# Row maxima subtracted on GpSimd, one exponential for a group of four blocks

## What is computed

```python
k_sum = k.reshape(B, H, nb, block, D).max(axis=3)      # block = 32, nb = 24
v_sum = v.reshape(B, H, nb, block, D).mean(axis=3)
scores_l = scale * np.matmul(q, k.transpose(0, 1, 3, 2))
mask_l = np.abs(pos[:, None] - pos[None, :]) < window   # window = 16
scores_s = scale * np.einsum('bhsd,bhnd->bhsn', q, k_sum) + np.log(block)
scores_all = np.concatenate([np.where(mask_l, scores_l, -1e9), scores_s], axis=-1)
scores_all = scores_all - np.max(scores_all, axis=-1, keepdims=True)
a = np.exp(scores_all)
a = a / (np.sum(a, axis=-1, keepdims=True) + 1e-09)
attn = np.matmul(a, np.concatenate([v, v_sum], axis=2))
```

## Time and profile before

| what | value |
|---|---|
| time, median of 3 runs | 504.31 us (503.15 to 505.6) |
| span of the profiled execution | 501.4 us |
| TensorE busy | 478.4 us (95%) |
| VectorE busy | 221.7 us (44%) |
| ScalarE busy | 191.6 us (38%) |
| GpSimd busy | 114.6 us (23%) |
| TensorE busy, 30 to 60 us | 25.52 of 30 us |
| ScalarE busy, 30 to 60 us | 27.21 of 30 us |

### The profile page before, as it was taken

One profiled execution on the slowest core, in us unless ns is written; L12 is line 12 of the kernel. 1 busy time (PEld: TensorE's weight loads), 2 busy tenths in 40 slices (PEclk: granted clock), 3 DMA queues, 4 the chain that ended last, 5 costly groups with the idle time before them and its releaser, 6 DMA issues.

```text
span 501.4 us, 8399 instructions
## 1 busy us (share of the span) xinstructions
PE 478.4 (95%) x2968; PEld 444.9 (89%) x2968; DVE 221.7 (44%) x575; ACT 191.6 (38%) x424; POOL 114.6 (23%) x98
## 2 busy tenths in 40 slices
PE   4798789998999999999999999999999999999996
PEld 4677678787999999999999999999889989989985
DVE  5598887499411141114111411456436355444521
ACT  3799887424211121112111211345455256353411
POOL 6364553285999000000000024300000000000000
PEclk9999999999999999999999999999999999999999
DMA  9999997144443100000000010000010001001001
GB/s 196 181 208 215 228 213 186 46 126 129 166 149 145 43 1 0 0 0 0 0 0 0 0 42 0 0 1 0 1 49 14 0 21 42 0 0 63 0 0 63
DMA packets 48657, 31.70 MB, mean 63 GB/s; under 512 B 21248, under 2 KB 42496, under 8 KB 48640
## 3 DMA queue, kind: packets, MB, share of 16 engines
q1 hardware_dynamic: 48640, 31.49, 26.4%
HBM read 27.14 MB, written 3.15 MB: 60 GB/s over the span
## 4 chain that ended last, share of the span: by engine, by line
PE 84%; SPq 5%; DMA 5%; ACT 2%; issue 2%; DVE 1%; POOL 0%; ACTq 0%; POOLq 0%
PE bank L946 26%; PE bank L947 26%; PE bank L948 26%; DMA kn<-in_k_dram 4%; SPq L301 2%; PE bank L998 1%; SPq L310 1%; DMA v<-in_v_dram 1%; PE bank L976 1%; ACT e_sb L518 1%; PE bank L1017 1%; ACT qbd L498 1%; PE bank L895 1%; SPq L321 1%; PE bank L928 1%
## 5 line engine op out<-in xcount | busy, mean ns | idle before, releaser
L845 DVE SCALAR_TENSOR_TENSOR rL<-bank,rH 128x384 fp32r<-128x384 f32 x48 | 26.7, 557 | 148.2 <-ACT rH L614 148.2
L614 ACT ACTIVATE rH<-bank 128x384 fp32r<-128x384 f32 x48 | 23.6, 492 | 163.1 <-PE bank L948 158.7
L946 PE MATMUL bank<-uH,W1H 128*128 128x384 f32 x192 | 64.8, 337 | 0.0
L947 PE MATMUL bank<-uL,W1H 128*128 128x384 f32 x192 | 64.6, 336 | 0.0
L948 PE MATMUL bank<-uH,W1L 128*128 128x384 f32 x192 | 64.4, 336 | 0.0
L947 PE MATMUL bank<-xkL,WkH 128*128 128x384 f32 x128 | 43.3, 338 | 0.0
L946 PE MATMUL bank<-xkH,WkH 128*128 128x384 f32 x128 | 43.1, 337 | 0.0
L948 PE MATMUL bank<-xkH,WkL 128*128 128x384 f32 x128 | 42.8, 335 | 0.0
L947 PEld LDWEIGHTS bank<-uL,W1H 128*128 128x128 f32 x192 | 36.1, 188 | 0.0
L948 PEld LDWEIGHTS bank<-uH,W1L 128*128 128x128 f32 x192 | 36.0, 188 | 0.0
L946 PEld LDWEIGHTS bank<-uH,W1H 128*128 128x128 f32 x192 | 36.0, 188 | 0.0
(11 more groups left out here) (131 smaller groups left out, 1093.2 us busy)
## 6 DMA issues: line engine op xcount, KB each, us to landing
stg<-in_moe_w_ch_dram SPq DMA_DIRECT2D x12, 512.0 KB, 3.6
vw<-in_v_dram SPq DMA_DIRECT2D x16, 240.0 KB, 4.9
kn<-in_k_dram SPq DMA_DIRECT2D x16, 192.0 KB, 3.8
qn<-in_q_dram SPq DMA_DIRECT2D x16, 192.0 KB, 4.4
v<-in_v_dram SPq DMA_DIRECT2D x16, 192.0 KB, 5.1
out_dram<-o_sb SPq DMA_DIRECT2D x12, 256.0 KB, 2.0
stg<-in_moe_w_k_dram SPq DMA_DIRECT2D x4, 512.0 KB, 3.5
stg<-in_moe_w_v_dram SPq DMA_DIRECT2D x4, 512.0 KB, 3.4
```

The costliest lines, as they stand in the source:

```text
L614: act.activation(rH[f % 2][:, :], bank[f % 2][:, 0:GR], ACT.Relu).then_inc(rh_done, 1)
L845: dve.scalar_tensor_tensor(out=rL[f % 2][:, :], in0=bank[f % 2][:, 0:GR], scalar=0.0, in1=rH[f % 2][:, :].bitcast(F32), op0=ALU.max, op1=A ...
L946: pe.matmul(dst, wH, mH, start=start, stop=False, **more)
L947: pe.matmul(dst, wH, mL, start=False, stop=False, **more)
```

## The change

GpSimd gets a new operation for each group, `below_max(G, r)`: it waits for the four maxima and subtracts `nmx`, spread over the 120 columns of each block, from `s_sb` in place. It raises `sub_done`. ScalarE waits for that and takes one exponential of 480 columns, without a bias. `exp_done` counts groups now. On GpSimd the three steps of `sum_values` are spread over the three groups of a pair, each behind that group's `below_max`; `split_x` of the pair before stands in group 1 and the low half of a weight (`low_wt`) at the end of group 2. The loop over pairs is written out.

```diff
+            def below_max(G, r):
+                pool.wait_ge(max_done, GU * G + GU)
+                pool.tensor_tensor(s_sb[r][:, :, :], s_sb[r][:, :, :],
+                                   nmx[:, r, :].unsqueeze(2).to_broadcast([P, GU, COLS]),
+                                   ALU.subtract).then_inc(sub_done, 1)
...
-            def pair(p, par, i=None):
-                if i is not None:
-                    sum_values(p + 2)
...
-                split_x(p)
+            def pair(p, par, i=None, earlier=True):
+                for r in range(NG):
+                    below_max(3 * p + r + 3, r)
+                    if i is not None:
+                        sum_values(p + 2, (r,))
+                    if r == 1 and earlier:
+                        split_x(p - 1)
+                    if i is not None and r == NG - 1:
+                        low_wt(p, par, i)
...
             sum_values(0)
+            below_max(0, 0)
+            below_max(1, 1)
             sum_values(1)
-            with pool.Fori(0, NP // 2 - 1) as i:
-                for par in range(2):
-                    pair(2 * i + par, par, i)
+            below_max(2, 2)
+            for p in range(NP - 2):
+                pair(p, p % 2, p // 2, p > 0)
             pair(NP - 2, 0)
+            split_x(NP - 2)
             split_x(NP - 1)
...
             def exps(G, r, par):
-                act.wait_ge(max_done, GU * G + GU)
-                for n in range(GU):
-
-                    act.activation(e_sb[par][:, n, :], s_sb[r][:, n, :], ACT.Exp, bias=nmx[:, r, n:n + 1],
-                                   scale=-1.0).then_inc(exp_done, 1)
+                act.wait_ge(sub_done, G + 1)
+                act.activation(e_sb[par][:, :, :], s_sb[r][:, :, :], ACT.Exp, scale=-1.0).then_inc(exp_done, 1)
```

More of the change, by code:

```diff
@@ L194, in build_program @@
         max_done = sem("max_done")
+        sub_done = sem("sub_done")
         exp_done, t_done, aT_done = sem("exp_done"), sem("t_done"), sem("aT_done")
@@ L431, in _ @@
                                pattern=[[-1, LOC]], channel_multiplier=0).then_inc(init_pool, 1)
[L433 to L441, removed]
@@ L443, in pair, with sum_values @@
-            def pair(p, par, i=None):
-                if i is not None:
-                    sum_values(p + 2)
[L446 to L452, removed]
-                split_x(p)
+            def sum_values(p, steps=(0, 1, 2)):
+                if 0 in steps:
+                    pool.wait_ge(ld_v8, 32 * p + 32)
+                    pool.tensor_tensor(v4[:, :, :, :], v8[:, :, 0:4, :], v8[:, :, 4:8, :],
+                                       ALU.add).then_inc(tree_step, 1)
+                if 1 in steps:
+                    pool.wait_ge(tree_step, 2 * p + 1)
+                    pool.tensor_tensor(v2[:, :, :, :], v4[:, :, 0:2, :], v4[:, :, 2:4, :],
+                                       ALU.add).then_inc(tree_step, 1)
+                if 2 in steps:
+                    pool.wait_ge(tree_step, 2 * p + 2)
+                    pool.wait_ge(vs_summed, p + 1)
+                    pool.tensor_tensor(v1[:, :, :], v2[:, :, 0, :], v2[:, :, 1, :], ALU.add).then_inc(v1_ready, 1)
@@ new lines, in below_max, with low_wt @@
+            def below_max(G, r):
[3 more added lines that the diff above has]
+                                   ALU.subtract).then_inc(sub_done, 1)
+            def low_wt(p, par, i):
+                pool.wait_ge(wh_done, p + 1)
+                if par == 0:
+                    hi, lo = wt1H[:, bass.ds(2 * i, 2), :], wt1L[:, bass.ds(2 * i, 2), :]
+                else:
+                    hi, lo = wt2H[:, :, bass.ds(TOK * i, TOK)], wt2L[:, :, bass.ds(TOK * i, TOK)]
+                pool.tensor_tensor(lo, halves(stg[par][:, 0:512]), hi.bitcast(F32),
+                                   ALU.subtract).then_inc(wl_done, 1)
@@ L765, in _ @@
                         if part == 0 or par == 0:
-                            maxima(G + 3, r, 1 - gp, GU * G + GU)
+                            maxima(G + 3, r, 1 - gp, G + 1)
                         if part == 1 and 3 * par + r == 2 * NG - 1:
@@ L973, in pair @@
                     G, gp = 3 * p + r, (3 * par + r) % 2
-                    pe.wait_ge(exp_done, GU * G + GU)
+                    pe.wait_ge(exp_done, G + 1)
                     for n in range(GU):
```

## The result

The changed kernel takes 539.14 us (median of 4 runs, 538.33 to 540.35), the one before 504.23 on the same chip: a ratio of 1.070, with a 95% interval from 1.067 to 1.072. The forecast was 529.5, the range 519 to 545. Ratios leave out executions more than 1.5% above the fastest of their kernel; of all kernels here only e8_wait_only had such, two of six.

The account below looks back on a forecast made before the run. No engine was full; attention was bound by a ring of pairs, 9.87 us each. Start 1.15, pair 0 4.1 and five pairs at 4.0 made 25.2 on 501.4: 526.6, or 529.5 beside the median; range 519 to 545.

Parts of the forecast that it names:

- The order: In the six prep pairs `v1` stands behind a subtraction on GpSimd, so TensorE waits 4 to 5 us before `sum_vs`.
- The pair: One steady attention pair, laid out with port waits: 13.85 us instead of 9.87, so 4.0 us more a pair.
- R: The start of `row_sums` of group 0 in a pair, from which the prediction counted its times.
- rival A: Attention: only the order costs, the port doesn't; 2.6 us a pair, 522 in all; chance 0.25 for 522 to 525.
- Pair 0 and the start: The first subtraction delays the start by 1.15 us; the group 2 output matmuls of pair 0 add 4.1.
- ScalarE: Attention: one 480-column exponential takes 0.6 us, saving 1.9 a pair, a gain only where ScalarE is waited for.
- Rival C: Attention: `v1` comes before TensorE asks, and freed ScalarE time gains 3 to 4 us, 500.5 in all; chance 0.03.
- the chain's share: The exponentials' part in the chain of waits of steady attention: 9.3% of 40 us, some 0.9 us a pair.
- rival B: TensorE's matmuls slow from the stall on: 2.5 us a pair, 544 in all; slow throughout, 555; chance 0.25.
- transposes of 1.5 for six: Sign of rival B: six transposes on TensorE taking 1.5 us, where 0.87 was measured in the steady part.
- The 2.9 us added to every span: Time outside the trace: the runs' median of 504.31 against a traced span of 501.4, added to every result.
- The port: VectorE and GpSimd lock each other out: `kw` copies stretch from 0.73 to 1.2 us, the summary-key copy to over 1.

Follow-up runs that it names:

- e8_wait_only: The kernel before with one wait added and nothing else: `v1` also waits for the maxima of group 2; 513.51 us, ratio 1.021.
- e1: The changed kernel with all three steps of the value sums behind the subtraction of group 0; 513.76 us, ratio 1.021.
- e7: The changed kernel with the value sums behind the subtraction of group 0 and `split_x` behind the low half of the weight in group 2; 506.69 us, ratio 1.008.
- e9: The kernel before with `v1` also waiting for the maxima of group 2, and 8 never-read matmuls filling TensorE's pause; 509.56 us, ratio 1.013.
- e5: The changed kernel with 19 never-read matmuls filling TensorE's pause before `sum_vs`; 527.2 us, ratio 1.048.
- e6: The changed kernel with `split_x` behind `v1` in group 2 and 12 never-read matmuls filling TensorE's pause; 518.28 us, ratio 1.031.
- e4: The kernel before with one exponential of 480 columns in place of four, the maxima made but not subtracted; 502.51 us, ratio 0.998.
- e2: The changed kernel with `split_x` moved from group 1 to behind `v1` in group 2; 527.56 us, ratio 1.048.

## Why the prediction was right

**The order.** As predicted, TensorE stands in front of `sum_vs` in each of the six prep pairs, 3.52 us in pair 0 and 5.16 in the others, where "4 to 5" was put. e1 and e7 take it away by moving the value sums ahead (e7 moves `split_x` too) and keep all the subtractions; e9 puts it in alone. This is shown.

**The pair.** The output matmuls of group 2 were put at 10.2 us from R; they are at 10.22. That match is luck, since errors of the working cancelled. The subtraction takes 0.99, not 1.2. The `kw` copy takes 2.58, not 1.24: `split_x` got the port ahead of it, the case that rival A gave 0.55 a pair more, and the summary-key copy, which I had waiting for `split_x` instead, takes its 0.29. And `sum_vs` runs at the low clock, 0.62 instead of 0.40; with the clock up, in e5, the output matmuls are at 9.83 from R. Pair 0 and the start were to cost 5.25 and cost 5.34, again by two errors: the first output matmuls are 1.9 us later than before (24.53 against 22.65) where 1.15 was put, and pair 0 adds 3.4 where 4.1 was. Without the clock a pair was to take 13.85, and e5 has 13.5; what follows the output matmuls up to the next R is 3.65 there, as forecast (62.06 to 65.71). A, order without port, was to take 12.5 a pair and 522; e6 has 12.0 and 518.

**ScalarE.** The exponential takes 0.6 us as estimated, and is not in the chain of waits of the changed kernel from 62 to 84 us. Rival C needed `v1` ahead of TensorE; e7 has that and is not faster, e4 shows that there was hardly anything to win. The 3 to 4 us that I gave C from the chain's share were too much: 0.998 is 1.1 us, the interval's end 2.2.

**The clock.** This is the step that failed in size. The forecast summed the pair at full clock and left the slow matmuls to rival B, with a chance of 0.25. B came true beside the forecast's own terms: its 2.5 us a pair are 2.4 (16.0 against 13.5 in e5). In the spans the sum reads so: the forecast added 25.2 us, and 37.2 were measured. Start and pair 0 are 0.1 above it, five pairs at full clock 1.6 below (13.5 for 13.85), and the clock, put at nothing, is 12.1 in the five pairs and 1.4 behind the last. B's 544 was thus nearer than the forecast, in mechanism and in number, and the number of 539 fell into the range because the range took in a part of B. B asked for "transposes of 1.5 for six" as its sign, and they are there: 1.48 at 37.14. The 2.9 us added to every span, a median less the span of one execution, were too much as well: the traced execution of the changed kernel took 540.35 us for a span of 538.6, 1.8 more.

The earlier trace rows held the sign for the clock. So did the Trainium skill's page "TensorE: Matmul & The Clock Gate", Part 1: an idle array falls to half clock. The traces agree: a granted clock of 0.50 behind each of the six pauses, output matmuls of 1.19 for 0.73 behind the longer five, and all of it gone when the pause is filled. The forecast took a rival's mechanism for an alternative to its own sum when it was another term of it, since the same pause brings both.

**The port.** The Trainium skill, "SBUF — State Buffer", "SBUF: two separate sides", has the holder keep the port for its whole instruction. The traces agree: the `kw` copy takes 0.73 alone, 0.93 when only the second value sum is in its way, 2.58 with `split_x`, and it ends 0.6 us after the instruction that it waited for.

## What to carry to other kernels

A piece of work that an in-order queue takes on stands in front of everything behind it: before moving an operation there, look for an instruction further back that a third engine waits for, and whether the new one's own input comes from that engine. Price a stall of TensorE twice, as the wait itself and as the slower clock behind it. Relieving an engine that is 90% busy gained nothing measurable here, where the ring passes through others; running the relief alone, with nothing paid for it, tells that in one run.

## What the runs showed of the hardware

**Who gets the port.** A VectorE copy that begins while GpSimd is in an instruction is passed by GpSimd's next one too, if that is ready: in the changed kernel, in e1 and in e7 the copy ended 0.6 us after the second GpSimd instruction, not after the first. Once in e1 it was passed by two: it began at 38.35 within `v1`, the subtraction and `split_x` went ahead of it, and it took 3.43 us. Where nothing is ready behind the first (e2), the copy is done 0.6 us after that one, in 0.93.

**How short a pause lowers the clock.** The clock fell at every pause of 5.16 us and every one of 3.5 us (the changed kernel and e2). At those of 5.16 us it was down before they ended, at those of 3.5 us it fell only after TensorE had started again, 0.3 to 1.2 us into the new work, so the first matmuls behind a pause can look fast and the price lie further on. Pauses of 2.37 us in the trace of e8 lowered it five times of six, and cost 0.7% in the executions that the ratios compare. What decides in a single short pause stays open.

**The subtraction.** 480 elements with an operand spread over 120 columns take 0.99 us on GpSimd, where 512 in a plain addition take 1.27. Whether the spread operand is the reason was not tried.
